# A recurrence stage on TensorE: 32 products with 64 columns of weights in place of 16 with 128

## The reference

```python
for t in range(S):
    y[:, :, t] = np.einsum('bhd,bhde->bhe', rt, state)
    Sa = np.einsum('bhde,bhe->bhd', state, at)
    state_decay = state * wt[:, :, None, :] - np.einsum('bhd,bhe->bhde', Sa, bt)
    state = state_decay + np.einsum('bhd,bhe->bhde', vt, kt)
```

## Time and profile before

| | us |
|---|---|
| median of 3 runs | 918.59 |
| lowest, highest | 911.92, 924.10 |
| the profiled execution | 923.58 |
| its span (first to last instruction) | 921.9 |
| the part with steps 0 to 17, within it | 75 to 332 |
| the end of the recurrence, within it | about 404 |

### The profile page before, as it was taken

The page is one execution under the profiler, slowest core; times in us unless marked ns, Lnnn a source line. Parts: engine busy times, 40 slices in busy tenths (PEclk is TensorE's granted clock), DMA queues, the critical chain, the costliest instruction groups (busy, mean ns, idle before and its releaser), DMA issues.

```text
span 921.9 us, 27713 instructions
## 1 busy us (share of the span) xinstructions
PE 824.6 (89%) x11872; PEld 597.0 (65%) x11872; DVE 559.7 (61%) x1235; ACT 317.4 (34%) x741; POOL 259.5 (28%) x525
## 2 busy tenths in 40 slices
PE   3428989998999988889998999988999998999988
PEld 3428889988998988864465654545644656545555
DVE  8995795878599742136528645357464277354474
ACT  4102331323133232222227542246432266322364
POOL 2087777778778877000000000000000000000000
PEclk9999895979599798899999999999999979999999
DMA  3645575657566574620100000100001000000000
GB/s 117 153 85 122 126 163 113 134 139 140 122 157 138 113 158 102 157 78 26 44 1 15 16 15 1 43 0 23 15 8 43 1 8 22 16 1 0 1 15 30
DMA packets 130922, 61.33 MB, mean 67 GB/s; under 512 B 106544, under 2 KB 119792, under 8 KB 130800
## 3 DMA queue, kind: packets, MB, share of 16 engines
q1 hardware_dynamic: 96156, 32.61, 16.3%
q10 hardware_dynamic: 34644, 26.95, 11.3%
HBM read 45.37 MB, written 14.16 MB: 65 GB/s over the span
## 4 chain that ended last, share of the span: by engine, by line
PE 75%; DVE 11%; issue 5%; ACT 5%; POOL 2%; DMA 1%; SPq 0%; ACTq 0%; DVEq 0%
PE ps_all L808 8%; PE ps_all L792 8%; PE ps_scan L105 5%; PE ps_all L852 5%; PE ps_scan L188 4%; PE ps_all L918 4%; PE ps_all L900 4%; PE ps_all L930 4%; PE ps_scan L130 3%; PE ps_scan L167 3%; PE ps_all L795 3%; PE ps_all L802 2%; PE ps_all L835 2%; PE ps_scan L122 2%; PE ps_scan L114 2%
## 5 line engine op out<-in xcount | busy, mean ns | idle before, releaser
L328 POOL TENSOR_TENSOR t_update<-solver_then_w_down 128x133 f32<-128x133 f32 (+13 forms) x251 | 118.6, 473 | 88.1 <-DMA solver_then_w_down<-l_blocks 39.1
L330 POOL TENSOR_TENSOR solver_then_w_down<-solver_then_w_down,t_update 128x133 f32<-128x133 f32 (+13 forms) x251 | 132.7, 529 | 19.7
L105 PE MATMUL ps_scan<-decayed_a_and_eye,scaled_then_x 40*128 40x104 f32 x768 | 67.6, 345 | 46.5 <-DVE decayed_a_and_eye L362 45.2
L1129 DVE TENSOR_REDUCE minus_max<-ps_all 128x1 f32<-128x128 f32 (+5 forms) x96 | 55.3, 617 | 66.8 <-PE ps_all L904 66.8
L105 PEld LDWEIGHTS ps_scan<-decayed_a_and_eye,scaled_then_x 40*128 40x128 f32 x768 | 62.8, 252 | 48.6 <-issue 47.7
L808 PE MATMUL ps_all<-gated,solver_then_w_down 128*128 128x384 f32 x256 | 91.1, 499 | 0.0
L792 PE MATMUL ps_all<-scaled_then_x,inputs_then_w_up 128*128 128x384 f32 x256 | 88.8, 490 | 1.8 <-ACT ak_l_then_ffn L970 1.8
L1028 ACT ACTIVATE probs_t<-ps_all 128x512 f32<-128x512 f32 (+3 forms) x128 | 55.1, 452 | 69.9 <-PE ps_all L918 69.3
L808 PEld LDWEIGHTS ps_all<-gated,solver_then_w_down 128*128 128x128 f32 x256 | 46.0, 189 | 44.6 <-issue 19.1
L792 PEld LDWEIGHTS ps_all<-scaled_then_x,inputs_then_w_up 128*128 128x128 f32 x256 | 47.6, 190 | 36.3 <-ACT ak_l_then_ffn L970 6.0
L232 ACT ACTIVATE x_rhs<-ps_scan 128x320 f32<-128x320 f32 x48 | 21.0, 438 | 141.3 <-PE ps_scan L122 70.5
(11 more groups left out here) (117 smaller groups left out, 1523.8 us busy)
## 6 DMA issues: line engine op xcount, KB each, us to landing
r_t_and_v_t<-in_rv ACTq DMA_DIRECT2D x48, 160.0 KB
inputs_then_w_up<-in_x ACTq DMA_DIRECT2D x46, 160.0 KB
solver_then_w_down<-l_blocks SPq DMA_DIRECT2D x22, 256.0 KB, 4.6
uv_and_ruv<-in_v ACTq DMA_DIRECT2D x48, 80.0 KB, 3.7
y_t<-y_out SPq DMA_DIRECT2D x24, 160.0 KB
out<-out_rows SPq DMA_DIRECT2D x24, 160.0 KB, 1.8
inputs_then_w_up<-in_x ACTq DMA_DIRECT2D x46, 81.4 KB
inputs_then_w_up<-in_x ACTq DMA_DIRECT2D x46, 80.0 KB
```

Of the source, the lines that this page charges most:

```text
L105: last = nc.tensor.matmul(PS[:, o:o + ROWS], weights, AL[c % NK][rows(h), p, :], start=True, stop=True)
L328: return (lambda: eng.tensor_tensor(tmp[:, 0:cols, 0:rest], l[:, s:s + 1, s + 1:BLK].broadcast_to(shape), t[:, 0:cols, s:s + 1].broadcast_ ...
L330: lambda: eng.tensor_tensor(t[:, 0:cols, s + 1:BLK], t[:, 0:cols, s + 1:BLK], tmp[:, 0:cols, 0:rest], ALU.subtract))
L1129: nc.vector.tensor_reduce(NM[:, v:v + 1], PS[:, first_bank(v) * 512:first_bank(v) * 512 + n], AX.X, ALU.min).then_inc(m["nm"], 1)
```

## The change

In g_products the product of one head, with all 128 columns of BK as weights, becomes two products of 64 columns each (j = 0, 1), which write the lower and the upper 64 partitions of the same place in PSUM. What is computed and where it lands stay the same. A step's stage L105 has 32 products in place of 16, in the order p, h, j. Nothing else is touched, the 236 extra waits included.

```diff
             for p in range(P8):
                 for h in range(2):
                     o = place(2 * h, p)
-                    weights = BK[c % 2][rows(h), p, :, :].rearrange("r j t -> r (j t)")
-                    last = nc.tensor.matmul(PS[:, o:o + ROWS], weights, AL[c % NK][rows(h), p, :], start=True, stop=True)
+                    for j in range(2):
+                        last = nc.tensor.matmul(PS[own(j), o:o + ROWS], BK[c % 2][rows(h), p, j, :], AL[c % NK][rows(h), p, :],
+                                                start=True, stop=True)
             last.then_inc(m["g"], 1)
```

## The result

The changed kernel took 924.03 us in the median of 20 runs (915.25 to 939.58), the kernel before 919.25 in as many (909.93 to 927.79). The ratio is 1.0061 with an interval of 1.0034 to 1.0088: 0.6% slower, some 5.6 us, which lies within the range of 906 to 933 around the predicted 919. All ratios in this document leave out executions that took over 1.5% longer than the fastest of their kernel. The two profiled executions, 923.58 and 924.02 us, do not show this difference; the profile has to show the mechanism and the runs the amount.

A forecast was written before the change was run, and what follows sets the result against it. TensorE was taken to bound the recurrence, with a floor of 3.65 to 4.0 us per packet of 256 instructions. 5.2 us lost less 4.4 gained made +0.8 us, so 919 us was predicted, range 906 to 933.

The forecast's parts named there:

- the two large terms: Full-clock steps lose 5.2 us to the instruction packets; six half-clock stages gain 4.4 us from the shorter L105.
- The sum, +0.8 us: Whole kernel: 5.2 us lost at full clock less 4.4 us gained at half clock.
- rival (b): Recurrence steps: late packets find no slack and TensorE's clock falls for one more stretch; up to 935 us, chance 0.16.
- I take L188's own time: Stage L105: 104 moving columns set its time, 0.41 us less a step at full clock, 0.74 at half.
- Four quarters side by side: Stage L105: 64 matmuls over two row and two column halves run in parallel, again 16 turns.
- Rival (c): Stage L105: products of one row half run one after the other, 3.12 us at full clock; 947 us, chance 0.04.
- nothing for the first five and 0.74 for the sixth: Six L105 stages before step 0: VectorE's work hides five, the sixth gains 0.74 us at half clock.
- I take +0.4 for each of the 13 full-clock steps: Full-clock steps: 3.25 packets under the floor make each 0.4 us longer, +5.2 us in all.
- steps that a late packet lengthens today stay as they are: Recurrence steps already lengthened by a late instruction packet: no change in their length.
- 3.65 to 4.0 us and never less: TensorE stretches of 256 instructions ending in a stop: this floor; any under 3.5 us would make the forecast wrong.
- Before, the floor costs little: Steps of the kernel before: only one short stretch of three, 3.0 us of work, lies well under the floor.
- rival (a): Recurrence steps: no packet floor holds, so the whole 9.8 us gain arrives; 909 us, chance 0.19.

The follow-up runs named there:

- experiment 4: Changed kernel with the four array quarters in alternating order, so no two products of one row half are neighbours; 1.0013, repeated 1.0145, of the kernel before.
- split_ahead: Kernel before with the new form only in the seven turns up to step 0, the old form in steps 1 to 17; 0.9937 of the kernel before.
- experiment 7: Changed kernel with loads of w, k, b and a cut to 8 columns per part from chunk 2 on; 0.9953 of the kernel before.
- experiment 6: Three kernels (before, half stage, changed) with solver steps 13 to 18 left out on GpSimd for pairs 2 to 11; 0.9847, 0.9907, 1.0044 of the kernel before.
- experiment 2: Changed kernel without the products for the upper 64 partitions (j = 0 alone), keeping 768 instructions a step; 0.9936 of the kernel before.
- old_plus_16: Kernel before with 16 small products ahead of the old stage in every g_products, 832 instructions a step; 1.0134 of the kernel before.
- one_half: The kernel of experiment 2: changed kernel with j = 0 alone, upper 64 partitions left out; 0.9936 of the kernel before.
- before_short: Kernel before with solver steps 13 to 18 left out on GpSimd for pairs 2 to 11; 0.9847 of the kernel before.
- one_half_short: one_half with solver steps 13 to 18 left out for pairs 2 to 11; 0.9907 of the kernel before, 1.006 of before_short.
- after_short: Changed kernel with solver steps 13 to 18 left out for pairs 2 to 11; 1.0044 of the kernel before, 1.020 of before_short.
- small_loads: The kernel of experiment 7: changed kernel with loads of 8 columns per part from chunk 2 on; 0.9953 of the kernel before.

## Why the prediction was right, and where it was not

**The forecast and its range.** No change was forecast, at 919 us, within 906 to 933; measured were 0.6% more. The direction of the two large terms was right and they nearly cancelled. The sum, +0.8 us, was short by some 5 us. That it came so near is partly luck: the stage gained more than was taken, the full-clock steps lost more, and the clock, a part of the outcome, stood in rival (b) only.

**The stage.** "I take L188's own time: 1.56 us at full clock, 2.93 us at half clock." It is 1.66 and 3.16 us from its first matmul to the next stage; with the sooner start the gains are 0.52 and 0.82 us. Four quarters side by side: right, since 64 matmuls take less time than 32 did. Rival (c), by which the stage would take 3 us at full clock, is refuted by the same rows; experiment 4 found nothing for it in the order of the quarters.

**The stages before step 0.** L105 of step 0 went from 75.02 to 74.25 us in the profiled execution, as nothing for the first five and 0.74 for the sixth had it. One execution each is thin: split_ahead, with the new form in the same turns, has 75.48 us.

**The cost at full clock.** "I take +0.4 for each of the 13 full-clock steps": this is the term that was mis-sized. The full-clock steps went from 12.0 to 12.6 us, +0.6, which was the mean of the bounds that the prediction had written down and then left ("3.25 x 3.88 = 12.6 us at the mean"). An estimate from these two executions is 13 x 0.2 = 2.6 us of the missing 5. Late packets, too, were taken as the same in both kernels ("steps that a late packet lengthens today stay as they are"). With 31 us of stops for 14 they did not stay, and experiment 7 makes fewer transfers worth some 10 us in the changed kernel. How that splits over the median can't be told from one profiled execution each.

**The floor.** "3.65 to 4.0 us and never less" failed. Stretches that end in a stop go down to 3.25 us in the changed kernel (237.71 to 240.96 us). There the transfer starts 0.3 us after the stretch does, while after a stop it never starts sooner than 1.0 us; the request may go out before the first instruction of the stretch runs, which no record shows. Where a stop stands at both ends the least length in all kept traces is 3.45 us, with others at 3.73 and 4.00. The kernel before had shorter ones too, which the four chosen rows did not show (260.15 to 263.27 us, 3.12). The prediction had named such a stretch as a sign that it is wrong; that sign was too strict, since a packet of 3.45 us still makes 11.2 us of 3.25 of them, over the 11.0 us of work.

**"Before, the floor costs little."** True of the kernel before as it is, but it hides how near the floor lies. By experiment 6 the full-clock steps got no shorter in the mean when the stage did and the instructions stayed 768. The prediction's loss was right for the changed kernel, and experiment 2 makes it unlikely that rival (a)'s 9.8 us were within reach even with free instructions: it gained 5.9.

**The half-clock steps and the clock.** In the profiled executions the half-clock steps kept their gain and there were fewer: the granted clock of the stretch rose from 0.86 to 0.90. Over all timed executions it is the other way round, as rival (b) had it. Mean time and mean granted clock of the executions behind the ratios, and the mean of their product, which is roughly the time that would be left at full clock:

| kernel | us | clock | product, us |
|---|---|---|---|
| before, four groups | 911.5 to 917.2 | 0.956 to 0.965 | 877 to 879 |
| changed, twice | 922.1 and 921.3 | 0.953 and 0.951 | 879 and 876 |
| old_plus_16 | 933.8 | 0.949 | 887 |
| one_half | 914.2 | 0.956 | 874 |
| before_short | 903.1 | 0.970 | 876 |
| one_half_short | 906.0 | 0.962 | 872 |
| after_short | 919.9 | 0.953 | 876 |
| small_loads | 913.0 | 0.954 | 871 |
| split_ahead | 911.7 | 0.962 | 877 |

In the product the changed kernel, before_short, after_short and split_ahead do not differ from the kernel before by more than its groups differ among themselves; in time before_short alone lies 12 us under the kernel before beside it, and the changed kernel 5 us and more over it. So by this estimate the gain of the stage and the cost of the packets did cancel, as the sum had it, and most of the missing 5 us is time at the lower clock. The profiled executions tie the clock to the stops: between 75 and 410 us it fell to half nine times in each kernel, and in 17 of the 18 cases a stop for instructions had begun in the 8 us before. It fell in or right after each of the changed kernel's four stops of over 3 us there. Many shorter stops are not followed by a fall. No run held the clock fixed, so this share is argued and not shown.

**Signs that came as said.** 64 matmuls a step, 100 packets, "issue" over 20 us and at ten lines, full-clock steps near 12.4 (12.6).

## What to carry to other kernels

Where a stage is cut into smaller matmuls, count the instructions first: in these traces a TensorE that had less than some 3.5 to 3.7 us of work in 256 of them was paced by the packets that bring them, whatever its array could do. The sign in a profile is "issue" before a matmul at borders 256 instructions apart, with one packet of the instruction queue between them. Such stops can cost twice, once by themselves and once by the granted clock after them, so the clock of every timed execution belongs beside its time. Finer products cost nothing that was seen where TensorE waits for others anyway, as in the turns before step 0 here.

## What the runs showed of the hardware that was not expected

- TensorE's stops for instructions between 75 and 335 us lie a multiple of 256 instructions apart in every kept trace, and in the changed kernel each ends 2.3 to 3.3 us after the start of a transfer of the instruction queue.
- The stretches with a stop at both ends have lengths in steps: 3.45, 3.73 and 4.00 us, in several kernels.
- TensorE's granted clock fell to half nine times between 75 and 410 us in each kernel, in 17 of the 18 cases within 8 us of the start of a stop for instructions.
- A product with 64 weight columns can start in the array among the last ones of the stage before: 0.84 us from first_blocks to L105 in place of 1.06.
- 128 small matmuls (40 weight columns, 4 moving) took 1.5 to 1.8 us where 1.1 was expected from their columns, and TensorE's granted clock was 0.79 over the stretch, though TensorE was busy for 295.6 of 316.8 us.
- Shortening the solver on GpSimd, for which ScalarE waited 3.7 us in one place, made the kernel before 14 us faster; in the profiled executions most of that came before the last two pairs (step 17 began at 309.6 us for 320.0). The granted clock went with it, 0.970 for 0.960 over the timed executions; why it was higher is open.
